# Decays, keys and receptance of a pair of heads loaded in one transfer of 128 rows instead of one per head

## The chip, the cores and the metric

The kernel runs on one core of a Trainium2 chip. Its engines are TensorE (PE, matrix products), VectorE (DVE), ScalarE (ACT), GpSimd (POOL) and SyncE (SP), which here only issues DMAs; 16 DMA engines carry the transfers. The metric is the time of the program on the device in microseconds, the median of several runs.

## The reference

Three parts follow one another. The first is a linear attention with decay, for 4 batches, 8 heads, 768 steps and a head width of 48. The second is a product of gated matrices without a nonlinearity, and the third a mixture of 8 experts, two for each token.

```python
for t in range(S):                                   # per batch and head
    cur = einsum('bhd,bhe->bhde', u[None] * k[t], v[t])
    y[t] = einsum('bhd,bhde->bhe', r[t], state + cur)
    state = w[t][:, None] * state + einsum('bhd,bhe->bhde', k[t], v[t])
x = y as [3072, 384]
x = ((x @ w1) * (x @ w2)) @ w3 @ w_out               # 384 -> 1024 -> 1024 -> 384
logits = x @ w_gate + log1p(exp(x @ w_noise)) * noise
out = sum over the two best experts e: weight * relu(x @ ew1[e]) @ ew2[e]
```

Everything is float32.

## The kernel before

**Stages.** The attention works on pairs of heads: 4 batches of 4 pairs, 16 in all, numbered g = 4 b + q. Three stages follow one another on every engine. In the opening (to about 106 us) the four pairs of batch 0 run, interleaved with the product of w3 and w_out (`w3_mm`: 8 rows of blocks, each with its own load of w3T, 512 KB) and with the preparation of w1 and w2 (loads of wraw, 512 KB, from which w12h and w12l are made). In the middle (to about 478 us) the fused layer of one batch runs beside the attention of the next, and behind it the experts with their own weights.

**A pair.** Its heads share the 128 partitions: head 0 lies in partitions 0 to 47, head 1 in 64 to 111. Rows 48 to 63 and 112 to 127 are fill, 1 for the decays and 0 for keys and receptance, so that every later step may work on all 128. The steps of a pair on DVE are the running product of the decays (`dve_decays`, L254, six scans of wt), its reciprocal (`dve_inverse`, L265, three times), the scaled keys (`dve_keys`, kt, L272) and queries (`dve_queries`, rt, L278), then ruk from the rows kn and rn (L289, L295) and its sums diag (L304). ACT spreads diag into att (L317). PE computes the scores in two halves (L186), turns the scaled keys (L195), forms the products for the state (L207) and the outputs (L231, L237). DVE masks each half of the scores (L325) and steps the state (L335).

**Loads.** All of them are issued by SP, in the order in which its program stands, and go through the same 16 DMA engines. Each tile wt, kt, rt, kn, rn, vs has two buffers. A pair's transposed inputs come from arrays that the host has laid out as [batch, head, 64, 768], already with the fill; `sp_input_load` (L140 to 148) loads one of the three tensors of a pair with two transfers, one for each head. For the first two pairs (g < 2), which fill the two buffers, a transfer has all 64 rows; from then on 48, since the fill rows stay in the buffer. A row has 768 values, 3,072 bytes. So a transfer has 192 KB or 144 KB. The semaphore `loaded` counts 16 per transfer, and DVE waits for 32 per pair. The rows kn and rn (288 KB each) and the values vs (384 KB: 128 rows of 3,072 bytes) have one transfer per pair already.

**The order around the loads.** In the opening SP first issues the loads of pairs 0 and 1 with w_out (two of 768 KB), w3T 0 and 1 and two of wraw between them; the rest follows the list of steps (`order`, made by `threaded`): the loads of pair g + 2 are issued in the place of the same step for pair g + 1, each behind a wait for the buffer (L144), the stores of the attention's output at `out` (L169, four per pair), vs behind them, and w3T n + 2 at the end of block row n (L526). The table of slots (slot_entry, 1,568 KB) is written after the first output of pair 1. PE waits at the first block of each row of w3T for its load (L682), and whatever stands behind this in its program, the second half of a pair's scores among them, waits too.

Of the kernel before, what the change touches and what calls it, by code (L numbers as in the profile page):

```python
# [5 lines left out]
B, H, S, D = 4, 8, 768, 48  # L6
# [8 lines left out]
HP = H // 2  # L15
HB = 64
# [29 lines left out]
def need(eng, sem, count):  # L46

    if not isinstance(count, int) or count > 0:
        eng.wait_ge(sem, count)
# [8 lines left out]
def program(nc, w_turned, k_turned, r_turned, k_rows, r_rows, v_rows, u, w1, w2, w3_turned, w_out, gate_rows, noise_rows, ew1, ew2_rows, out):  # L58
# [10 lines left out]
    with top:  # L69
# [34 lines left out]
        wt, kt, rt = ([asb(f"{x}t{i}", [P, S]) for i in range(2)] for x in "wkr")  # L104
# [19 lines left out]
        loaded = [[sem(f"{x}_loaded{i}") for i in range(2)] for x in "wkr"]  # L124
# [15 lines left out]

        def sp_input_load(sp, b, q, n):
            g, i = HP * b + q, q % 2
            rows = HB if g < 2 else D
            need(sp, (decay_ready, kdiv_ready, rdec_ready)[n], g - 1)  # L144
            for h in range(2):
                sp.dma_start((wt, kt, rt)[n][i][h * HB:h * HB + rows, :],
                             (w_turned, k_turned, r_turned)[n][bass.ds(b, 1), 2 * q + h, 0:rows, :].rearrange("o d t -> (o d) t")
                             ).then_inc(loaded[n][i], 16)

        def sp_rows_load(sp, b, q):  # L150
            g, i = HP * b + q, q % 2
# [96 lines left out]
        def dve_decays(dve, b, q):  # L248

            g = HP * b + q  # L250
            dve.wait_ge(loaded[0][q % 2], 32 * (2 * b + q // 2 + 1))
            need(dve, state_ready, (NC - 1) * (g - 1))
            for c in range(NC):
                last = nc.vector.tensor_tensor_scan(decay[q % 2][:, c, 1:C + 1], wt[q % 2][:, c * C:(c + 1) * C],  # L254
                                                    wt[q % 2][:, c * C:(c + 1) * C], 1.0, ALU.mult, ALU.bypass)
            last.then_inc(decay_ready, 1)
# [10 lines left out]

        def dve_keys(dve, b, q):
            g = HP * b + q
            dve.wait_ge(loaded[1][q % 2], 32 * (2 * b + q // 2 + 1))  # L270
            dve.wait_ge(inverse_ready, 3 * (g + 1))
            nc.vector.tensor_tensor(kdiv[q % 2][:, :], kt[q % 2][:, :], kdiv[q % 2][:, :], ALU.mult).then_inc(kdiv_ready, 1)  # L272

        def dve_queries(dve, b, q):
            g = HP * b + q
            dve.wait_ge(loaded[2][q % 2], 32 * (2 * b + q // 2 + 1))
            need(dve, yu_full, 3 * (g - 1))
            nc.vector.tensor_tensor(rdec[q % 2][:, :].rearrange("p (c x) -> p c x", c=NC),  # L278
                                    rt[q % 2][:, :].rearrange("p (c x) -> p c x", c=NC), decay[q % 2][:, :, 0:C],
                                    ALU.mult).then_inc(rdec_ready, 1)  # L280
# [169 lines left out]
        def sp_attention(sp, b, step, q, n):  # L450

            if later(b, q) is None:
                return
            after = later(b, q + 2)
            b, q = later(b, q)
            g = HP * b + q
            if step == "out":
                sp_attention_store(sp, b, q, n)
                if n == 1 and after:
                    sp_values_load(sp, *after)  # L460
            elif not after:
                return
            elif step == "derive" and n in (0, 4, 5):
                sp_input_load(sp, *after, max(0, n - 3))
            elif step == "diag" and n == 0:
                sp_rows_load(sp, *after)
# [31 lines left out]
        with ExitStack() as ph:  # L498
# [24 lines left out]
            def first_sp(sp):  # L523
# [4 lines left out]
                def load_w12(n):  # L528
# [3 lines left out]
                    sp.dma_start(wraw[n % 2][:, :], (w1, w2)[m][kk * P:(kk + 1) * P, :]).then_inc(wraw_loaded[n % 2], 16)  # L532

                sp_input_load(sp, 0, 0, 0)
                for part in range(2):
                    sp.dma_start(wo[:, 4 * part:4 * part + 4, 0:DM],
# [1147 lines left out]
def laid_out(np, inputs):  # L1684

    a = {name: np.asarray(x) for name, x in inputs.items()}

    def turned(x, fill):
        return np.pad(x.transpose(0, 1, 3, 2), [(0, 0), (0, 0), (0, HB - D), (0, 0)], constant_values=fill)

    def rows(x, pad):
        x = x.reshape(B, HP, 2, NC, P, D).transpose(0, 1, 4, 3, 2, 5)
        return np.pad(x, [(0, 0)] * 5 + [(0, pad)])

    return {
        "w": turned(a["w"], 1), "k": turned(a["k"], 0), "r": turned(a["r"], 0),
        "k_rows": rows(a["k"], 0), "r_rows": rows(a["r"], 0), "v_rows": rows(a["v"], HB - D), "u": a["u"],
        "moe_w1": a["moe_w1"], "moe_w2": a["moe_w2"],
        "moe_w3": a["moe_w3"].reshape(KF, P, KF, P).transpose(0, 3, 2, 1).reshape(KF, P, F1),
        "moe_w_out": a["moe_w_out"],  # L1700
        "gates": np.concatenate([a["moe2_w_gate"], a["moe2_w_noise"]], axis=1).reshape(KD, P, 2 * E).transpose(1, 0, 2),
        "moe2_noise": a["moe2_noise"].reshape(NT, P, E).transpose(1, 0, 2),
        "moe2_w1": a["moe2_w1"],
        "moe2_w2": a["moe2_w2"].reshape(E, KF // 2, 2, P, DM).transpose(0, 1, 3, 2, 4),
    }
# [17 lines left out]
```

## Time and profile before

| | us |
|---|---|
| median of 3 runs | 997.93 (997.01 to 1000.2) |
| the profiled execution, own time | 993.22 |
| its span, first to last instruction | 991.5 |
| PE busy | 951.2 (96%) |
| DVE busy | 676.3 (68%) |
| ACT busy | 528.1 (53%) |
| SP's hardware queue, share of the 16 DMA engines | 50.7% |
| mean granted clock of TensorE | 0.99 of full speed |

Busy times are those of the span. In a table of windows the columns are: the stretch, its length, busy time and instructions of PE, PE's weight loads, DVE, ACT and POOL, then the granted clock, the busy share of the DMA engines and the GB/s that they moved. In a timeline they are start, busy time, engine, line, operation, output and inputs, count, and in brackets the idle time before it with its releaser. SPq is SP's queue of DMA issues: the time there is that of the issue, not of the transfer.

### The profile page before, as it was taken

Reading aid. Unit: us, or ns where it says so; the run is one execution under the profiler, and the core shown is the slowest. Engines: PE = TensorE matmul, PEld = TensorE weight load, DVE = VectorE, ACT = ScalarE, POOL = GpSimd, SP = SyncE. Lnnn points to the kernel's source line nnn. Section 1 sums busy time; section 2 is a strip of 40 time slices with the busy share of each in tenths; the row PEclk is TensorE's granted clock in tenths of the full one; section 3 lists DMA queues with packets and bytes.
Section 4 is the critical chain, followed back from the end, with each engine's and each line's share of the span. In section 5 each row is a group of like instructions: output and inputs, shape, how many; then the busy total and the mean of one; then the engine's idle time right before and its main releaser. Section 6 shows DMA issues by size and latency. Waiting matters only on the chain.

```text
span 991.5 us, 18086 instructions
## 1 busy us (share of the span) xinstructions
PE 951.2 (96%) x6825; PEld 895.8 (90%) x6825; DVE 676.3 (68%) x1133; ACT 528.1 (53%) x986; POOL 221.3 (22%) x209
## 2 busy tenths in 40 slices
PE   5799999999999999999989999999999999999995
PEld 3455899999999999999989999999999999999995
DVE  5688886969696966256766685656856558566570
ACT  3354454555454645325644575655756557565560
POOL 0000000020202020221443323344232432324311
PEclk9889999999999999999999999999999999999998
DMA  9968434353435121216548797877968779787751
GB/s 262 295 190 263 142 85 143 105 160 95 143 106 172 57 71 41 81 52 217 177 123 244 196 294 214 241 257 205 308 206 243 262 202 301 211 245 258 212 152 17
DMA packets 93771, 179.61 MB, mean 181 GB/s; under 512 B 19042, under 2 KB 50532, under 8 KB 93684
## 3 DMA queue, kind: packets, MB, share of 16 engines
q1 hardware_dynamic: 80308, 157.77, 50.7%
q0 software_dynamic: 12976, 20.66, 10.1%
q8 instruction: 54, 0.88, 0.4%
q14 instruction: 33, 0.27, 0.1%
q10 hardware_dynamic: 400, 0.02, 0.0%
HBM read 152.81 MB, written 26.97 MB: 181 GB/s over the span
## 4 chain that ended last, share of the span: by engine, by line
PE 86%; DVE 3%; DMA 3%; ACT 2%; SPq 2%; issue 2%; another core or an unknown queue 0%; POOL 0%; DVEq 0%; ACTq 0%; POOLq 0%
PE pp L1233 20%; PE bank L1217 19%; PE bank L788 13%; PE bank L805 7%; PE fx L788 6%; PE fx L805 4%; PE yu L1276 3%; PE pp L186 2%; DMA w3T<-in_moe_w 2%; PE tr L1198 2%; PE yu L1258 1%; PE fx L1258 1%; PE yu L207 1%; PE yu L237 1%; DMA rn<-in_r_rows 1%
## 5 line engine op out<-in xcount | busy, mean ns | idle before, releaser
L1127 POOL DMA_INDIRECT result<-x2s,who x55 | 92.4, 1681 | 292.5 <-ACT x2s L1350 279.6
L1337 DVE SCALAR_TENSOR_TENSOR abl<-bank,abh 128x512 fp32r<-128x512 f32 x96 | 66.2, 691 | 113.7 <-ACT abh L1332 90.0
L978 POOL DMA_INDIRECT slot_entry<-entry,slot_i x48 | 52.1, 1086 | 334.6 <-DVE token_f L967 322.4
L1217 PE MATMUL bank<-xh,set_up_h 128*128 128x256 f32 x384 | 109.2, 284 | 0.0
L1217 PE MATMUL bank<-xh,set_up_l 128*128 128x256 f32 x384 | 108.6, 283 | 0.0
L1217 PE MATMUL bank<-xl,set_up_h 128*128 128x256 f32 x384 | 108.6, 283 | 0.0
L1332 ACT ACTIVATE abh<-bank 128x512 fp32r<-128x512 f32 x96 | 57.5, 599 | 85.1 <-PE bank L1217 80.2
L788 PE MATMUL bank<-xh,w12h 128*128 128x384 f32 x264 | 89.5, 339 | 1.0 <-DVE xl L485 0.9
L788 PE MATMUL bank<-xh,w12l 128*128 128x384 f32 x264 | 88.4, 335 | 0.0
L788 PE MATMUL bank<-xl,w12h 128*128 128x384 f32 x264 | 88.2, 334 | 0.0
L1233 PE MATMUL pp<-set_down_h,abh 128*128 128x384 f32 x256 | 87.7, 342 | 0.0
L1233 PE MATMUL pp<-set_down_h,abl 128*128 128x384 f32 x256 | 85.7, 335 | 0.0
L1233 PE MATMUL pp<-set_down_l,abh 128*128 128x384 f32 x256 | 85.6, 334 | 0.0
L265 DVE RECIPROCAL kdiv<-decay 128x256 f32<-128x256 f32 x48 | 82.2, 1734 | 0.3
L1114 POOL DMA_INDIRECT tokens<-ffn_out,who x55 | 72.6, 1319 | 32.9 <-issue 23.3
L1217 PEld LDWEIGHTS bank<-xh,set_up_h 128*128 128x128 f32 x384 | 73.5, 191 | 0.5 <-DVE abl L1337 0.2
L1217 PEld LDWEIGHTS bank<-xl,set_up_h 128*128 128x128 f32 x384 | 73.5, 192 | 0.3
L1217 PEld LDWEIGHTS bank<-xh,set_up_l 128*128 128x128 f32 x384 | 73.5, 191 | 0.0
L1350 ACT ACTIVATE x2s<-pp,who 128x384 f32<-128x384 f32 x48 | 28.0, 582 | 84.3 <-PE pp L1233 75.5
L317 ACT ACTIVATE att<-ident,diag 128x128 f32<-128x128 f32 x192 | 59.4, 389 | 15.0 <-DVE diag L304 15.0
L1305 DVE TENSOR_TENSOR set_up_l<-up_raw,set_up_h 128x1024 fp32r<-128x1024 f32 x48 | 57.6, 1224 | 9.3 <-ACT set_up_h L1300 8.8
L1305 DVE TENSOR_TENSOR w12l<-up_raw,w12h 128x1024 fp32r<-128x1024 f32 x45 | 55.0, 1223 | 8.5 <-ACT w12h L1300 5.6
(254 smaller groups left out, 2646.2 us busy)
## 6 DMA issues: line engine op xcount, KB each, us to landing
up_raw<-in_moe_w SPq DMA_DIRECT2D x93, 512.0 KB
down_raw<-in_moe_w SPq DMA_DIRECT2D x124, 384.0 KB
vs<-in_v_rows SPq DMA_DIRECT2D x16, 384.0 KB, 3.6
kn<-in_k_rows SPq DMA_DIRECT2D x16, 288.0 KB, 3.6
rn<-in_r_rows SPq DMA_DIRECT2D x16, 288.0 KB, 4.8
attention_out<-yt SPq DMA_DIRECT2D x64, 72.0 KB, 2.0
result<-zeros SPq DMA_DIRECT2D x12, 384.0 KB
ffn_out<-x2s SPq DMA_DIRECT2D x8, 576.0 KB
```

The source lines that it names most:

```text
L265: nc.vector.reciprocal(kdiv[q % 2][:, :].rearrange("p (c x) -> p c x", c=NC)[:, two, :], decay[q % 2][:, two, 1:C + 1]).then_inc(inverse_r ...
L317: last = nc.scalar.activation(att[:, j, h, c, :], ident[:, :], ACT.Copy, scale=diag[:, 3 * j + c, h:h + 1])
L788: last = nc.tensor.matmul(half_bank[n % 3][:, 0:TG], wp[:, m, kk, f * P:(f + 1) * P], xp[:, kk, :], start=(p == 0), stop=(p == 3 * KD - 1))
L805: last = nc.tensor.matmul(sum_at[s][:, 0:WA], xp[:, f, s * P:(s + 1) * P], wp[:, f, :], start=(f == 0 and n == 0), stop=(f == KF - 1 and n ...
L978: nc.gpsimd.indirect_dma_start(slot_entry, bass.IndirectOffsetOnAxis(slot_i[:, s, n:n + 1], 0), entry[:, s, n, :], None).then_inc(scattere ...
L1114: nc.gpsimd.indirect_dma_start(xg[v % 2][:, s, :], None, stored, bass.IndirectOffsetOnAxis(who[v % 4][:, s, 0:1], 0)).then_inc(gathered[v ...
L1127: nc.gpsimd.indirect_dma_start(out, bass.IndirectOffsetOnAxis(who[v % 4][:, s, 0:1], 0), yo[v % 2][:, s, 0:DM], None, bounds_check=N - 1, ...
L1217: last = nc.tensor.matmul(bank[m % 2][:, f * T2:(f + 1) * T2], wp[:, kk, c:c + P], xp[:, kk, :], start=(n == 0), stop=(n == 3 * KD - 1))
L1233: last = nc.tensor.matmul(pp[:, s, 0:DM], xp[:, f, s * P:(s + 1) * P], wp[:, f, :], start=(f == 0 and n == 0), stop=(f == KF - 1 and n == 2))
L1305: nc.vector.tensor_tensor(low, src, high.bitcast(f32), ALU.subtract).then_inc(w_low, 1)
L1332: nc.scalar.activation(hh[:, 2 * m:2 * m + 2, :].rearrange("p a t -> p (a t)"), bank[m % 2][:, :], ACT.Relu).then_inc(hh_ready, 1)
L1337: nc.vector.scalar_tensor_tensor(hl[:, 2 * m:2 * m + 2, :].rearrange("p a t -> p (a t)"), bank[m % 2][:, :], 0.0, hh[:, 2 * m:2 * m + 2, : ...
```

## The change

`sp_input_load` issues one transfer for a tensor of a pair: all 128 rows, for every pair. The host's arrays are the same bytes, seen as [batch, pair, 128, 768], so that the two heads and their fill lie in one piece. DVE waits for 16 per pair instead of 32. For the 14 pairs from g = 2 on each tensor's transfer carries 32 more rows, 98,304 bytes; for the first two pairs the bytes are the same.

```diff
         def sp_input_load(sp, b, q, n):
             g, i = HP * b + q, q % 2
-            rows = HB if g < 2 else D
             need(sp, (decay_ready, kdiv_ready, rdec_ready)[n], g - 1)
-            for h in range(2):
-                sp.dma_start((wt, kt, rt)[n][i][h * HB:h * HB + rows, :],
-                             (w_turned, k_turned, r_turned)[n][bass.ds(b, 1), 2 * q + h, 0:rows, :].rearrange("o d t -> (o d) t")
-                             ).then_inc(loaded[n][i], 16)
+            sp.dma_start((wt, kt, rt)[n][i][:, :],
+                         (w_turned, k_turned, r_turned)[n][bass.ds(b, 1), q, :, :].rearrange("o x t -> (o x) t")
+                         ).then_inc(loaded[n][i], 16)
...
         def dve_decays(dve, b, q):
-            dve.wait_ge(loaded[0][q % 2], 32 * (2 * b + q // 2 + 1))
+            dve.wait_ge(loaded[0][q % 2], 16 * (2 * b + q // 2 + 1))
...
         def dve_keys(dve, b, q):
-            dve.wait_ge(loaded[1][q % 2], 32 * (2 * b + q // 2 + 1))
+            dve.wait_ge(loaded[1][q % 2], 16 * (2 * b + q // 2 + 1))
...
         def dve_queries(dve, b, q):
-            dve.wait_ge(loaded[2][q % 2], 32 * (2 * b + q // 2 + 1))
+            dve.wait_ge(loaded[2][q % 2], 16 * (2 * b + q // 2 + 1))
...
     def turned(x, fill):
-        return np.pad(x.transpose(0, 1, 3, 2), [(0, 0), (0, 0), (0, HB - D), (0, 0)], constant_values=fill)
+        x = np.pad(x.transpose(0, 1, 3, 2), [(0, 0), (0, 0), (0, HB - D), (0, 0)], constant_values=fill)
+        return x.reshape(B, HP, 2 * HB, S)
```

No engine's instructions change their order. On SP, from its second issue to the loads of pair 0's rows, this stands in a row before (partitions x elements, x how many):

```order
L146 DMA wt<-in_w 64x768 x2
L536 DMA wo<-in_moe_w_out 128x4x384 x2
L146 DMA kt<-in_k 64x768 x2
L146 DMA rt<-in_r 64x768 x2
L526 DMA w3T<-in_moe_w 128x1024
L154 DMA kn<-in_k_rows 128x576
L154 DMA rn<-in_r_rows 128x576
```

and this now:

```order
L144 DMA wt<-in_w 128x768
L534 DMA wo<-in_moe_w_out 128x4x384 x2
L144 DMA kt<-in_k 128x768
L144 DMA rt<-in_r 128x768
L524 DMA w3T<-in_moe_w 128x1024
L152 DMA kn<-in_k_rows 128x576
L152 DMA rn<-in_r_rows 128x576
```

Three issues fewer stand ahead of rn, with the same bytes. Further on in SP's program, from the loads of pair 2 to the third load of w3T, this stands before:

```order
L146 DMA wt<-in_w 48x768 x2
L146 DMA kt<-in_k 48x768 x2
L146 DMA rt<-in_r 48x768 x2
L154 DMA kn<-in_k_rows 128x576
L154 DMA rn<-in_r_rows 128x576
L146 DMA wt<-in_w 48x768 x2
L154 DMA kn<-in_k_rows 128x576
L154 DMA rn<-in_r_rows 128x576
L169 DMA attention_out<-yt 48x3x128 x4
L161 DMA vs<-in_v_rows 128x768
L526 DMA w3T<-in_moe_w 128x1024
```

and this now:

```order
L144 DMA wt<-in_w 128x768
L144 DMA kt<-in_k 128x768
L144 DMA rt<-in_r 128x768
L152 DMA kn<-in_k_rows 128x576
L152 DMA rn<-in_r_rows 128x576
L144 DMA wt<-in_w 128x768
L152 DMA kn<-in_k_rows 128x576
L152 DMA rn<-in_r_rows 128x576
L167 DMA attention_out<-yt 48x3x128 x4
L159 DMA vs<-in_v_rows 128x768
L524 DMA w3T<-in_moe_w 128x1024
```

Four of the loads there (three of pair 2, the decays of pair 3) are one issue instead of two and carry 128 rows instead of twice 48.

## Rows read from the trace of the kernel before

**Rows 1.** The page: tenths in 40 slices, PE busy and granted clock
```profile
PE   5799999999999999999989999999999999999995
PEclk9889999999999999999999999999999999999998
```

**Rows 2.** Windows: the opening, the middle, and a stretch within the opening
```profile
0.00:106.00 106.00, 82.14 (x568) 51.28 (x568) 78.66 (x115) 48.35 (x121) 4.16 (x51) 0.94 0.84 244
106.00:478.00 372.00, 371.29 (x2825) 353.61 (x2826) 273.74 (x612) 180.57 (x448) 42.90 (x40) 1.00 0.37 111
...
55.00:65.00 10.00, 9.79 (x65) 5.67 (x63) 9.97 (x12) 5.01 (x14) 0.00 (x0) 0.95 0.52 157
```

**Rows 3.** The chain that ended last, opening: start us, us, what
```profile
7.79 10.19 DMA rn<-in_r_rows
...
35.99 10.29 DMA w3T<-in_moe_w
...
70.48 10.28 DMA w3T<-in_moe_w
```

**Rows 4.** DMA issues, the w3T issued at 88.63: KB, us to landing
```profile
w3T<-in_moe_w SPq DMA_DIRECT2D x1, 512.0 KB, 5.6
```

**Rows 5.** Windows: stretches in which transfers of one form pass
```profile
26.00:29.50 3.50, 3.50 (x36) 2.03 (x36) 3.36 (x11) 1.46 (x5) 0.00 (x0) 1.00 1.02 404
...
9.00:12.50 3.50, 2.83 (x12) 2.21 (x12) 3.50 (x3) 1.76 (x3) 0.00 (x0) 1.00 1.05 219
18.50:23.50 5.00, 3.71 (x33) 2.23 (x25) 3.04 (x5) 3.44 (x12) 0.00 (x0) 1.00 1.05 234
29.50:34.00 4.50, 4.50 (x32) 2.88 (x27) 4.47 (x5) 1.45 (x3) 0.00 (x0) 1.00 1.05 208
```

**Rows 6.** Windows: the same with their tails, and the slow clock
```profile
9.00:14.50 5.50, 4.73 (x21) 3.88 (x22) 4.05 (x4) 2.35 (x4) 0.00 (x0) 1.00 1.03 241
18.50:26.00 7.50, 5.86 (x65) 4.00 (x58) 4.16 (x7) 5.01 (x16) 0.00 (x0) 1.00 1.04 245
...
29.50:38.00 8.50, 8.03 (x42) 4.59 (x36) 8.36 (x9) 4.95 (x13) 0.00 (x0) 1.00 1.05 224
...
42.50:56.00 13.50, 9.69 (x42) 5.87 (x43) 4.26 (x12) 2.84 (x7) 0.00 (x0) 0.50 0.59 166
```

**Rows 7.** Timeline of SP's issues: the first, and two groups of four stores
```profile
0.82 1.22 SPq L146 DMA_DIRECT2D wt<-in_w  x2
...
32.29 3.17 SPq L169 DMA_DIRECT2D attention_out<-yt  x4
...
118.05 1.81 SPq L169 DMA_DIRECT2D attention_out<-yt  x4
```

**Rows 8.** Timeline, ACT: the first spreads of diag
```profile
20.44 3.62 ACT L317 ACTIVATE att<-ident,diag 128x128 f32<-128x128 f32 x12 [1.23 <-DVE diag L304]
```

**Rows 9.** Timeline, PE and DVE: around the two waits for w3T
```profile
39.50 0.77 PE L195 MATMUL tr<-ident,kdiv 128*128 128x128 f32 x5
...
46.31 3.04 PE L682 MATMUL fx<-wo,w3T 128*128 128x400 f32 x4 [6.05 <-DMA w3T<-in_moe_w]
...
51.05 1.01 DVE L325 COPY_PREDICATED att<-causal,pp 128x768 f32<-128x768 int32 x1 [9.24 <-PE pp L186]
...
52.61 1.18 DVE L335 SCALAR_TENSOR_TENSOR added<-added,decay 128x48 f32<-128x48 f32 x4 [0.55 <-ACT added L341]
...
66.89 1.51 PE L682 MATMUL bank<-wo,w3T 128*128 128x400 f32 x4
...
69.38 1.01 DVE L325 COPY_PREDICATED att<-causal,pp 128x768 f32<-128x768 int32 x1 [1.26 <-PE pp L186]
...
70.42 1.18 DVE L335 SCALAR_TENSOR_TENSOR added<-added,decay 128x48 f32<-128x48 f32 x4
...
80.80 4.30 PE L682 MATMUL bank<-wo,w3T 128*128 128x400 f32 x12 [1.35 <-DMA w3T<-in_moe_w]
...
82.66 0.95 DVE L278 TENSOR_TENSOR rdec<-rt,decay 128x768 f32<-128x768 f32 x1
```

## The prediction

> **What bounds the kernel now.** I read the page first, for the stage that can move. Of 40 slices TensorE (PE) has a busy digit below 9 only in the first two and in the last, and the granted clock has its 8s in the second and third [rows 1]. The table by stage says it in us: from 106 to 478 PE works 371.29 of 372.00 us, in the first 106 only 82.14, with the DMA engines at a share of 0.84 [rows 2]. Behind 478 nothing of the change is left, and between 106 and 478 its loads are issued two pairs ahead of their use, with the DMA engines at 0.37, under a full PE: there I cost the change at nothing. Its cover is that distance, some 50 us, against transfers of under 2 us. So the question is the opening.
>
> The chain of waits runs there through three landings: rn, 10.19 us to 17.98, a w3T, 10.29 us to 46.27, and another, 10.28 us to 80.75 [rows 3]. PE stood 6.05 and 1.35 us for these two w3T, and VectorE (DVE) 9.24 us for the scores that PE computes behind the first [rows 9]. A load of 512 KB that takes 10.3 us, where one issued at 88.63 takes 5.6 [rows 4], stands in a queue. So the next view is the rate of the DMA engines in the stretches that the order of SP's issues lets me name. All 16 are at a share of about 1 in each of the stretches, yet move very different amounts: 404 GB/s in 26.0:29.5, where wraw, vs and wraw pass, all of 128 rows; 219 in 9.0:12.5 (kt and rt of pair 0, halves of 64 rows), 234 in 18.5:23.5 (pair 1), 208 in 29.5:34.0 (pair 2, halves of 48 rows) [rows 5]. Which transfers pass is read by adding up the bytes that SP issues, in its order, against what the engines moved. A half at a time moves at about half speed: that is what the opening pays.
>
> **The change, part by part.** *Rate.* The new transfer is 128 rows of 3,072 bytes in one piece, exactly the form of vs, so I take 404 GB/s. The Trainium skill speaks against that figure: DMA: Bandwidth & Descriptors, "Where 436 GB/s comes from", says that a load from HBM is bound at some 358 GB/s on the HBM side. This trace disagrees (404 GB/s over 3.5 us, [rows 5]); by the page a transfer would take 1.10 us and not 0.97, and the ten ahead of the first w3T 1.3 us more, which the slack of 3 us found below would swallow. The skill's page SBUF — State Buffer, "Can I just issue two DMAs to hit both halves?", gives two concurrent halves only 6% more than one half; if instead they did fill both sides, the merge would save nothing, and the rows (208 to 234 against 404) side with the page.
>
> *Time of the DMA engines ahead of the w3T that PE waits for.* I cut the busy stretches around the slow transfers, with the tail in which they still hold engines up [rows 6], and refill them at 404 GB/s. 9.0:14.5 holds 241 x 5.5 = 1.33 MB: 3.3 us instead of 5.5, saves 2.2. 18.5:26.0 holds 1.84 MB: 4.6 instead of 7.5, saves 2.9. 29.5:38.0 holds 1.90 MB, and four transfers in it (three of pair 2, the decays of pair 3) now carry 32 more rows each, 0.098 MB, in all 0.39: 2.30 MB take 5.7 instead of 8.5, saves 2.8. For the first one, in the start-up, I take 0.9: one issue of 0.6 us falls away ahead of its landing ([rows 7]: two take 1.22), and of its 0.393 MB the rate saves up to 0.393/219 - 0.393/404 = 0.8, of which I count 0.3, as the start-up limits it too. Sum 8.8 us: what was through at 38 is through by 29 or so, before SP issues more.
>
> *A, the start of the chain.* Decays start 0.9 earlier, and rn, for which DVE waits, lands 0.9 + 2.2 = 3.1 earlier, so diag could be ready 3.1 us sooner. ScalarE's spreads, which wait for it, start at 20.44 after an idle time of 1.23 [rows 8]: their engine is free at 19.21, after gates_side, which hangs on wo and moves by the 0.9 only. So they start at 18.3, and the chain gains 2.1 us. Bounds: 1.2 (wo does not move) to 3.1 (all of rn).
>
> *B, the stall for w3T.* Its issue stands behind four stores, which took 3.17 us in the crowded queue and 1.81 in a free one [rows 7]: issue at 35.99 - 2.1 - 1.4 = 32.5. With the queue nearly empty it lands 5.6 us later, or up to 1.3 more with vs and the stores before it: 38.1 to 39.4, I take 38.8. PE is ready for it when its key transposes end (39.50 + 0.77, less 2.1: 38.2) [rows 9]. The wait of 6.05 becomes 0.6: 5.45 us. Bounds 3.0 (as much again queued) to 6.05.
>
> *C, the clock.* From 42.5 to 56 the granted clock is 0.50, the lower of the two levels, after PE had been idle since 40.27 [rows 6, 9]; the pause of 1.35 us before 80.80 saw no fall (the fourth digit is 9, [rows 1]). With a pause of 0.6 us I expect none. From w3T's first matmul to DVE's mask of the second scores the slow stretch took 51.05 - 46.31 = 4.74 us, the same steps at full clock 69.38 - 66.89 = 2.49; from there to DVE's state step 1.56 against 1.04 [rows 9]. Saves 2.25 + 0.5 = 2.8. PE's later matmuls there gain too, but DVE is then busy without a gap to 65 us (9.97 of 10 us from 55) [rows 2] and sets the pace. Bounds 0 to 2.8.
>
> *D, the second stall.* PE waits 1.35 us at 80.80 for w3T. Ahead of it lie kt and rt of pair 4 (two issues fewer, about 1 us of SP; about 0.6 us each of the DMA engines) and the table of slots, which starts earlier. The wait goes; next in line is DVE's rdec (82.66 + 0.95 = 83.6, [rows 9]), so PE's scores, which follow the twelve matmuls begun at 80.80, can move by those 1.3 us and not by more. Bounds 0 to 1.4.
>
> Sum: 2.1 + 5.45 + 2.8 + 1.3 = 11.7 us. From 85 on DVE and PE run as before and carry it to the end. The profiled run goes from 993.22 to 981.5 (span 991.5 to 979.8). The median of the runs, 997.93, lies 4.7 above the profiled run; I take the same 11.7 off it: **986.2**. About 0.3% (3.0 us) is what a measurement of this kernel can tell from no change.
>
> **The rivals.** *The clock falls anyway, or w3T still comes late.* Without C the gain is 8.9 (989.0); with B at its low end too, A at 1.2 and D at 0 it is 4.2 (993.7). For it: w3T's issue hangs on SP's waits, and PE had little to do ahead of it. Against: the queue is empty by then, by 3 us and more. 0.24.
>
> *Hidden anyway.* DVE, busy 78.66 of 106 us, takes over where PE's waits go, or the transfers' rate is set by something that vs escapes and the gain is no more than the saved issues (A at 1.2, and some of the stores' 1.4): 995 to 998. Against: DVE's own largest idle time, 9.24 us at 51.05, is the same stall. 0.07.
>
> *Slower: more bytes at the old rate.* If the merged transfer moved at 208 GB/s, each filled one would cost 0.098 MB / 208 = 0.47 us more: four ahead of the first w3T 1.9, two ahead of the one at 80.75 another 0.95, in all 2.8: 1000.8. It decides below 277 GB/s, where 0.393 MB take as long as 0.295 MB now at 208. For it: only that no row shows this very tensor in 128 rows. Against: vs, whose form it is. 0.03.
>
> *More than summed*: the stalls at 37.5 and 69.4, where PE and DVE pass work back and forth, shrink as well, over 14 us, under 984: 0.03.
>
> **How the numbers follow.** The forecast (9 to 14 us gained) has 0.63. Faster by over 0.3%: 0.63 + 0.24 + 0.03 = 0.90; within 0.3%: 0.07; slower 0.03. The range runs from the sum of the upper ends (13.3, and 0.9 for the spread of the runs: 983.7) to the late end of the first rival, 993.7, and 0.8 more: 983.5 to 994.5; it leaves out the last three cases.
>
> **What would show it.** Right: DMA stretches around kt and rt at 350 GB/s or more; a busy DMA stretch that ends some us before w3T is issued at 32 to 34, landing in under 7 us; no wait over 2 us of PE for w3T; granted clock 1.00 from 42 to 56; the step to the fused layer's first matmul (105.97 now) near 94; the stages behind it as long as before. Wrong: 128-row loads of w, k, r under 277 GB/s; w3T landing after 41; a clock of 0.50 in spite of a short wait; or a stretch behind 106 that is longer by the extra 2.9 MB.

## The result and the profile after

| | before | after |
|---|---|---|
| median of 4 runs, us | 997.47 (993.61 to 1000.2) | 982.92 (980.96 to 983.7) |
| ratio, 95% interval | | 0.9854 (0.9818 to 0.9890) |
| profiled execution, own time | 993.22 | 980.96 |
| its span | 991.5 | 979.2 |
| first matmul of the fused layer (end of the opening) | 105.97 | 93.70 |

The kernel is 14.6 us faster by the medians and 12.3 us by the profiled executions. The forecast said 986.2 in a range from 983.5 to 994.5; the direction, the place and the profiled execution came out (981.5 forecast, 980.96 measured), the median lies 0.6 us under the range.

The page of the kernel after, beside [rows 1], tenths in 40 slices:

```profile
PE   6989999999999999999989999999999999999995
...
PEclk9999999999999999999999999999999999999998
```

The table of windows of the kernel after, by stage, beside [rows 2]:

```profile
0.00:93.70 93.70, 78.75 (x568) 49.75 (x568) 78.51 (x115) 48.34 (x121) 4.16 (x51) 0.96 0.85 291
93.70:465.70 372.00, 371.25 (x2824) 353.57 (x2825) 273.75 (x611) 180.52 (x448) 42.81 (x40) 1.00 0.38 119
465.70:979.20 513.50, 497.81 (x3436) 491.02 (x3434) 323.89 (x408) 299.17 (x418) 175.79 (x118) 0.99 0.74 219
```

Only the first row has changed its length, by 12.27 us. VectorE (DVE) is busy there for 78.5 us, where it was for 78.7; TensorE (PE) for 78.75 instead of 82.14 with the same 568 instructions, at a mean granted clock of 0.96 instead of 0.94. The other two rows are as long as before to 0.1 us, with 119 instead of 111 GB/s in the middle: the 2.9 MB more cost nothing there.

The rates, beside [rows 5]: windows of the kernel after in which kt and rt of pair 0 pass, and those of pairs 1 and 2 among others:

```profile
7.00:9.50 2.50, 2.50 (x13) 2.08 (x13) 2.50 (x2) 1.21 (x3) 0.00 (x0) 1.00 1.06 396
14.00:20.00 6.00, 4.31 (x35) 2.89 (x35) 2.92 (x5) 3.98 (x14) 0.00 (x0) 1.00 1.03 411
26.00:29.00 3.00, 3.00 (x47) 2.36 (x40) 2.97 (x4) 0.96 (x2) 0.00 (x0) 1.00 1.06 401
```

The stretches of 208 to 234 GB/s around these loads are gone; in the three windows the engines move 396 to 411. (Not everything does: in 29.5:34.0 of the kernel after, where the four stores of the attention's output, 48 partitions each, pass with kn, rn and vs, it is 320 GB/s.) From here on w3T 2 is the third load of w3T, the one that PE stood 6.05 us for; the spreads are ScalarE's (ACT's) first ones of diag. The timeline of the kernel after at the places of [rows 8, 9] (start, busy us, in brackets the idle time before):

```profile
6.55 5.12 PE L656 MATMUL bank<-ident,wo 128*128 128x128 f32 x24 [6.55 <-DMA wo<-in_moe_w_out]
...
16.31 3.62 ACT L315 ACTIVATE att<-ident,diag 128x128 f32<-128x128 f32 x12 [2.02 <-DVE diag L302]
...
35.83 0.77 PE L193 MATMUL tr<-ident,kdiv 128*128 128x128 f32 x5
36.43 1.51 PE L680 MATMUL fx<-wo,w3T 128*128 128x400 f32 x4
...
38.93 1.02 DVE L323 COPY_PREDICATED att<-causal,pp 128x768 f32<-128x768 int32 x1 [0.77 <-PE pp L184]
39.97 1.18 DVE L333 SCALAR_TENSOR_TENSOR added<-added,decay 128x48 f32<-128x48 f32 x4
...
56.74 1.02 DVE L323 COPY_PREDICATED att<-causal,pp 128x768 f32<-128x768 int32 x1 [1.26 <-PE pp L184]
57.78 1.18 DVE L333 SCALAR_TENSOR_TENSOR added<-added,decay 128x48 f32<-128x48 f32 x4
...
71.07 0.94 PE L184 MATMUL pp<-rdec,kdiv 48*128 48x128 f32 x12 [1.67 <-DVE kdiv L270]
...
77.76 1.18 DVE L333 SCALAR_TENSOR_TENSOR added<-added,decay 128x48 f32<-128x48 f32 x4
```

PE's wait of 6.05 us for w3T at 46.31 has become none: 36.43 follows straight on the key transposes that begin at 35.83. DVE's wait of 9.24 us for the second scores is 0.77. By DVE's state steps the gain over the kernel before is 3.9 us at the first pair (25.91 to 22.04), 12.6 at the second (52.61 to 39.97) and third (70.42 to 57.78), 14.0 at the scores of the fourth (85.03 to 71.07), and 12.3 at its state step (90.03 to 77.76), where it stays. The rows of before for the first and the last three of these, which stand in no group above:

```profile
25.91 1.18 DVE L335 SCALAR_TENSOR_TENSOR added<-added,decay 128x48 f32<-128x48 f32 x4 [0.43 <-ACT added L341]
...
85.03 0.94 PE L186 MATMUL pp<-rdec,kdiv 48*128 48x128 f32 x12
...
90.03 1.18 DVE L335 SCALAR_TENSOR_TENSOR added<-added,decay 128x48 f32<-128x48 f32 x4
```

The clock in the kernel after:

```profile
20.50:24.50 4.00, 3.94 (x25) 2.56 (x26) 3.20 (x10) 1.91 (x7) 0.00 (x0) 0.57 1.03 405
72.50:75.50 3.00, 3.00 (x8) 1.47 (x6) 1.27 (x2) 0.69 (x1) 0.00 (x0) 0.50 0.61 187
```

The long stretch at the lower level behind the stall (13.5 us, [rows 6]) is gone, but there are two short ones where the kernel before had none. The second lies between the two places at which the gain is 14.0 and 12.3; the 1.7 us between them are put down to it, as PE's five transposes and four matmuls, 0.77 and 1.51 us at full clock (35.83 and 36.43), take 1.22 and 2.79 there (71.94 and 72.95), together 1.7 more.

### The profile page after: what moved, and what is told of

Its sections match the earlier page's. It is cut to its first block, busy times and chain, and to the rows that moved or that the text cites. A ratio compares the mean times of both kernels' runs of the same rounds, so it can differ in the third digit from the quotient of the medians.

```text
span 979.2 us, 18038 instructions
## 1 busy us (share of the span) xinstructions
PE 947.8 (97%) x6825; PEld 894.3 (91%) x6825; DVE 676.2 (69%) x1133; ACT 528.0 (54%) x986; POOL 222.8 (23%) x209
## 3 DMA queue, kind: packets, MB, share of 16 engines
q0 software_dynamic: 12976, 20.66, 10.2%
## 4 chain that ended last, share of the span: by engine, by line
PE 87%; DVE 5%; ACT 3%; issue 2%; DMA 1%; SPq 0%; another core or an unknown queue 0%; POOL 0%; DVEq 0%; ACTq 0%; POOLq 0%
PE pp L1231 20%; PE bank L1215 20%; PE bank L786 13%; PE bank L803 7%; PE fx L786 6%; PE fx L803 4%; PE yu L1274 3%; PE pp L184 3%; PE tr L1196 2%; PE yu L1256 1%; PE fx L1256 1%; PE yu L205 1%; PE yu L235 1%; PE tr L193 1%; DVE kdiv L263 1%
## 5 line engine op out<-in xcount | busy, mean ns | idle before, releaser
L1125 POOL DMA_INDIRECT result<-x2s,who x55 | 92.5, 1681 | 290.3 <-ACT x2s L1348 277.4
L1335 DVE SCALAR_TENSOR_TENSOR abl<-bank,abh 128x512 fp32r<-128x512 f32 x96 | 66.2, 691 | 113.7 <-ACT abh L1330 97.5
```

The costliest lines, as they stand in the source:

```text
L1125: nc.gpsimd.indirect_dma_start(out, bass.IndirectOffsetOnAxis(who[v % 4][:, s, 0:1], 0), yo[v % 2][:, s, 0:DM], None, bounds_check=N - 1, ...
L1335: nc.vector.scalar_tensor_tensor(hl[:, 2 * m:2 * m + 2, :].rearrange("p a t -> p (a t)"), bank[m % 2][:, :], 0.0, hh[:, 2 * m:2 * m + 2, : ...
```

## The experiments

The experiments ran on four chips (4, 5, 12 and 14; that of the first comparison is not on record). Each is compared with runs of the kernel before on its own chip; the start of the expert stage differs from chip to chip (below), so spans are not compared across chips, but openings are.

**What makes the rate: bytes, number, size or partitions?** Two kernels have the bytes of the kernel after in two transfers per tensor. One takes the halves of the kernel before:

```diff
-            sp.dma_start((wt, kt, rt)[n][i][:, :],
-                         (w_turned, k_turned, r_turned)[n][bass.ds(b, 1), q, :, :].rearrange("o x t -> (o x) t")
-                         ).then_inc(loaded[n][i], 16)
+            for h in range(2):
+                sp.dma_start((wt, kt, rt)[n][i][h * HB:(h + 1) * HB, :],
+                             (w_turned, k_turned, r_turned)[n][bass.ds(b, 1), q, h * HB:(h + 1) * HB, :].rearrange("o x t -> (o x) t")
+                             ).then_inc(loaded[n][i], 16)
```

> The kernel after, but each tensor of a pair again in two transfers, rows 0 to 63 and rows 64 to 127, for every pair: the bytes of the kernel after, the number and the halves of the kernel before. Theory (a transfer to one half of the partitions moves at about half the rate): DMA rate around kt and rt of pair 0 near 220 GB/s, w3T 2 lands as late as before or later (46 to 49 us), PE waits 6 us or more for it, the fused layer's first matmul at 106 to 109 us, time 997 to 1001. Rival (the gain comes from something else, such as the layout of the host's arrays or the count of waits): opening ends near 94, time near 983.

The other takes the even rows to the even partitions and the odd ones to the odd:

```diff
-                sp.dma_start((wt, kt, rt)[n][i][h * HB:(h + 1) * HB, :],
-                             (w_turned, k_turned, r_turned)[n][bass.ds(b, 1), q, h * HB:(h + 1) * HB, :].rearrange("o x t -> (o x) t")
+                sp.dma_start((wt, kt, rt)[n][i][h:P:2, :],
+                             (w_turned, k_turned, r_turned)[n][bass.ds(b, 1), q, h:P:2, :].rearrange("o x t -> (o x) t")
```

> As the run with two halves, but one transfer has the even rows and partitions and the other the odd ones: still two issues of 64 rows and 192 KB per tensor, the same bytes, but each transfer spreads over all partitions. Theory (what counts is which partitions one transfer reaches): rate around kt and rt of pair 0 at 350 to 410 GB/s, first matmul of the fused layer at 94 to 97 us (the extra issues cost up to 2 us of SP at the start), time 982 to 987. By the Trainium skill, SBUF - State Buffer, section on the DMA port swizzle, even and odd partitions reach all 16 ports each, which points the same way. Rival (what counts is that the transfer is large and in one piece of DRAM, or that there are fewer issues): rate near 220, opening as before (106), time 997 to 1000.

Measured, with halves: 994.91 us, ratio 1.0030 (1.0004 to 1.0056), opening 111.1 us. Interleaved: 979.58 us, ratio 0.9867 (0.9844 to 0.9890), opening 96.2. Windows around the loads of pairs 0 and 1, halves first:

```profile
10.00:13.00 3.00, 2.72 (x12) 2.10 (x11) 2.41 (x2) 1.41 (x3) 0.00 (x0) 1.00 1.05 239
20.00:24.50 4.50, 2.13 (x7) 0.68 (x4) 2.44 (x5) 2.40 (x9) 0.00 (x0) 0.89 1.03 226
```

and interleaved:

```profile
9.00:12.00 3.00, 1.78 (x9) 1.59 (x9) 2.38 (x2) 0.58 (x1) 0.00 (x0) 1.00 1.03 402
16.00:20.00 4.00, 3.03 (x41) 1.92 (x42) 2.47 (x4) 1.46 (x5) 0.00 (x0) 1.00 1.03 411
```

PE's wait for w3T with halves:

```profile
52.52 3.03 PE L681 MATMUL fx<-wo,w3T 128*128 128x400 f32 x4 [9.74 <-DMA w3T<-in_moe_w]
```

Bytes, number of transfers and size are the same in both; what differs is which rows a transfer takes, and with them its partitions, and the rate goes from 226 to 239 GB/s to 402 to 411. It is neither the single transfer nor one contiguous piece of DRAM: the interleaved transfers read every other row. The two were not tried apart: no run sends the same rows of DRAM to other partitions. That the partitions decide is the reading that fits. The Trainium skill, SBUF — State Buffer, "Door 1: The DMA port swizzle (why `[64,N]` ≈ `[32,N]`)", lets partitions 0 to 63 reach 8 of 16 ports at some 218 GB/s; the windows with halves, in which other loads pass too, lie a little above at 226 to 239. The same page of the Trainium skill, in "Can I just issue two DMAs to hit both halves?", holds that "the only way to hit all 16 ports is one transfer spanning all 128 partitions". The runs part from it if that is read as all 128 in one: transfers of 64 partitions each, spread over both sides, come to 402 to 411 GB/s here. The run with halves is also nearly the slower rival of the prediction, made real (with two issues where the rival has one): the fill rows at the old rate cost 0.30%, 3.0 us, where 2.8 was worked out. The interval of that cost goes from 0.4 to 5.6 us, so its sign is shown and its size is not.

The openings came as expected with interleaved rows (94 to 97) and longer than expected with halves (106 to 109; w3T 2 landed at 52.5, not at 46 to 49). Both times lie below what was expected, 997 to 1001 and 982 to 987: the kernel before takes 992.62 on chip 5, 5 us less than in the first comparison. One thing stays unexplained: with interleaved rows w_out lands later than in the kernel before (PE's first transpose at 10.22 instead of 8.95), although the decays ahead of it are in 1.1 us sooner (their second transfer at 4.25 instead of 5.36 us) and SP issues w_out at the same time.

**Which of the loads pay?** The form of the load is chosen by pair (MERGED is the condition; the waits count 16 or 32 for each pair accordingly):

```diff
+            if MERGED(g):
                 sp.dma_start((wt, kt, rt)[n][i][:, :],
...
+            else:
+                for h in range(2):
+                    sp.dma_start((wt, kt, rt)[n][i][h * HB:h * HB + rows, :],
```

Pairs 0 and 1 merged, the others with 48 rows a head:

> One transfer of 128 rows for the first two pairs only, where it carries the same bytes; from the third pair on two of 48 rows as in the kernel before. Theory: nearly the whole gain at the start (ScalarE's first spreads at 16.3 to 17 us instead of 20.4), but pair 2 and the decays of pair 3 again take 1.5 us each of the DMA engines; since those were through at 29 with a margin, w3T 2 still lands within 2 us of when PE wants it. First matmul of the fused layer at 94 to 97, time 983 to 986. Rival (each of the ten transfers ahead of w3T 2 is needed): w3T 2 is waited for by 2 to 4 us and the clock falls long: 988 to 992.

Pairs 0 and 1 in halves of 64 rows, the others merged:

> Two transfers of 64 rows for the first two pairs, one of 128 from the third pair on. Theory: the start stays as before (ScalarE's first spreads at 20.4 us), the DMA queue is 2.8 us shorter ahead of w3T 2, which lands at 42 to 44 instead of 46.3; PE waits 2 to 4 us for it; the clock falls or not. First matmul of the fused layer at 99 to 103, time 990 to 995. Rival (the stall depends only on the large transfers behind): no change from the kernel before, 997.

Merged from pair 6 on only:

> One transfer of 128 rows only from the seventh pair on, whose loads are issued at the end of the opening and in the middle stage; the first six pairs as in the kernel before (64 and 48 rows a head). Theory: nothing, the middle stage runs at the pace of TensorE; its length stays within 0.5 us of 372, opening ends where that of the kernel before does (104 to 109 us), ratio 1.000 within its interval. Rival (2.9 MB more in the middle stage cost, or faster loads there gain): 1 us or more either way in the middle stage.

| merged | median, us | ratio (interval) | first spreads | wait for w3T 2 | end of opening |
|---|---|---|---|---|---|
| pairs 0, 1 | 980.85 | 0.9883 (0.9857 to 0.9909) | 16.39 | 3.06 | 96.9 |
| from pair 2 | 986.68 | 0.9956 (0.9925 to 0.9987) | 20.54 | 0.35 | 100.8 |
| from pair 6 | 990.92 | 0.9994 (0.9970 to 1.0018) | 20.81 | 5.64 | 107.0 |

PE's wait for w3T 2 in the timeline of the first of the three:

```profile
39.27 3.04 PE L690 MATMUL fx<-wo,w3T 128*128 128x400 f32 x4 [3.06 <-DMA w3T<-in_moe_w]
```

of the second:

```profile
41.87 1.61 PE L690 MATMUL fx<-wo,w3T 128*128 128x400 f32 x4 [0.35 <-DMA w3T<-in_moe_w]
```

and of the third:

```profile
46.28 3.04 PE L690 MATMUL fx<-wo,w3T 128*128 128x400 f32 x4 [5.64 <-DMA w3T<-in_moe_w]
```

Merging the first two pairs moves the start of the chain by 4 us and leaves a wait of 3.06 us, as the rival said and not the theory; the clock fell in it, but only for some 7 us (36.5 to 43.5), and the opening ends where the theory had it. The time lies below both, 983 to 986 and 988 to 992. Merging from the third on leaves the start as it was and takes nearly the whole stall, where 2 to 4 us were expected to stay; the opening came as expected (99 to 103), the time below it (990 to 995). There w3T 2 is issued at 35.99 as in the kernel before and lands in 5.84 us instead of 10.29: 4.4 us saved where the sum had 2.8 for the four transfers ahead of it. Whether the rest comes from kt and rt of pair 3, which follow right behind w3T and are merged too, was not tried apart. By the ratios the first two pairs alone take 1.17%, the others alone 0.44%, together 1.6 where the whole change gives 1.47: within the intervals they add up, though both act on the same stall. From pair 6 on the form is worth nothing that shows: in the middle stage PE works 371.3 of 372 us as before. That cost at nothing held.

**Why did the start gain 4.1 us and not 2.1?** PE's first transpose, which waits for w_out, moved by 2.4 us instead of 0.9. The rows of before:

```profile
8.95 2.88 PE L658 MATMUL bank<-ident,wo 128*128 128x128 f32 x12 [8.95 <-DMA wo<-in_moe_w_out]
12.60 2.91 PE L658 MATMUL bank<-ident,wo 128*128 128x128 f32 x12 [0.77 <-DMA wo<-in_moe_w_out]
```

Keys and receptance of pair 0, which are issued behind w_out, again in two halves of 64 rows, all else as in the kernel after:

```diff
+def MERGED(g, n):
+    return g > 0 or n == 0
```

> The kernel after, but keys and receptance of pair 0, and they alone, in two transfers of 64 rows. They are issued behind w_out. The prediction moved w_out by 0.9 us, it moved by 2.4 (PE's first transpose from 8.95 to 6.55 us). Theory 1 (slow transfers issued behind another hold up its landing): the first transpose starts at 7.5 us or later although nothing ahead of w_out differs from the kernel after, and the second half of the transposes has a gap again. Theory 2 (it is the decays ahead of w_out alone): first transpose at 6.5 us, 24 transposes without a gap to 11.7. In both, rn lands 2 us later than in the kernel after and the spreads start at 17.5 to 18.5 us.

```profile
6.63 4.30 PE L666 MATMUL bank<-ident,wo 128*128 128x128 f32 x20 [6.63 <-DMA wo<-in_moe_w_out]
11.10 0.65 PE L666 MATMUL bank<-ident,wo 128*128 128x128 f32 x4 [0.17 <-ACT woT L590]
```

984.13 us, ratio 0.9861 (0.9827 to 0.9895), spreads at 17.54. The second theory holds for the landing that the first transpose waits for: with the decays in one transfer and the slow ones behind, the first of w_out's two transfers lands at 6.49 us, in the kernel after at 6.41. The second lands 0.6 us later (9.22 instead of 8.61), which PE does not feel. In every profile with the decays in one transfer the first transpose comes at 6.5 to 7.3 us, in every one with two at 8.5 to 10.2.

What it is in the decays is not shown. Their rate it can't be alone: the run with interleaved rows has them in at the full rate, in two transfers, and has the latest w_out of all:

```profile
10.22 5.58 PE L657 MATMUL bank<-ident,wo 128*128 128x128 f32 x24 [10.22 <-DMA wo<-in_moe_w_out]
```

One issue instead of two lets SP issue w_out at 1.27 instead of 2.08 us, 0.8 of the 2.4; the rest is that its first transfer then takes 5.1 us to land instead of 6.7. The spreads come 1.2 us later than in the kernel after since rn lands later (ruk starts at 15.17 instead of 13.44); the expected start of 17.5 to 18.5 holds. The opening ends at 96.4, 3 us later than in the kernel after on that chip, with three falls of the clock (at 17, 54.5 and 75 us); the medians differ by 1.0 us.

**Does filling PE's waits keep the clock up?**

```diff
             if j == 0:
+                if 2 <= g < HP:
+                    pe.wait_ge(tr_free, g)
+                    for c in range(8):
+                        nc.tensor.transpose(tr[:, c // 4, (c % 4) * C:(c % 4 + 1) * C], ident[:, :], ident[:, :])
                 pe.wait_ge(kdiv_ready, g + 1)
```

> The kernel after with eight more transposes of the identity on TensorE ahead of its wait for the keys of pairs 2 and 3, into a PSUM tile that is overwritten next (work that nobody needs, some 1.1 us in a wait of 1.7 to 2.5 us). Theory: the half clock at 72.5 to 75.5 us in the kernel after follows the waits around 69 to 71 us, and cost 1.7 us between the scores of pair 3 (gain over before 14.0 at 71.07, 12.3 at 77.8): with the engine busy there the clock stays at 1.00 and the fused layer starts at 92 to 92.5 us, 1.2 to 1.7 us earlier. Rival (the falls come whatever the engine does in those waits): a fall at the same place, start at 93.7 or later.

982.94 us, beside 983.15 for the kernel after on the same chip. The opening lies between what the theory (92 to 92.5) and the rival (93.7 or later) had. There is no fall at 72, but one at 53.5, and one in the expert stage that this profile has and the kernel after's has not, the first row here, beside the kernel after on the same chip, the second:

```profile
495.19:525.19 30.00, 27.06 (x190) 26.65 (x189) 19.97 (x28) 14.87 (x21) 14.15 (x10) 0.94 0.68 172
```

```profile
495.43:525.43 30.00, 27.10 (x197) 26.70 (x196) 22.53 (x32) 17.61 (x25) 13.21 (x9) 1.00 0.75 201
```

Opening 93.2 against 93.4. That filling these waits avoids a fall is not shown, nor that it moved this one: a third profile of the unchanged kernel has no fall at 72 either. Over three profiles of the kernel after the falls lie at 20.5 and 72.0, at 71.5, and at 52.5 us: executions of one kernel differ in them.

**Can the start be shortened further?** In the kernel after DVE waits 0.54 us for the vector u of the reference (u_all), and the spreads for what follows. w3T 0 is issued behind kn, rn and u instead of ahead of them:

```diff
-                load_w3(0)
                 sp_rows_load(sp, 0, 0)
                 sp.dma_start(u_all[:, :, :, :].rearrange("p q h d -> p (q h d)"),
                              bass.AP(u.tensor, u.offset, [[0, P], [1, H * D]])).then_inc(small_loaded, 16)
+                load_w3(0)
```

> The kernel after with w3T 0 issued behind kn, rn and u of pair 0 instead of ahead of them. In the kernel after VectorE waits 0.54 us for u, and ScalarE's spreads wait 2.0 us for the diag that follows. Theory: rn and u land 1.3 us earlier (524 KB at 400 GB/s), spreads start at 15.5 to 15.7 instead of 16.3, w3T 0 lands before TensorE wants it at 16.6; opening ends 0.6 to 0.8 us earlier unless the clock falls elsewhere, time about 0.7 us under the kernel after. Rival (w3T 0 now comes late, or a fall of the clock eats it): same time or up to 1 us longer.

978.05 us beside 976.77 for the kernel after on the same chip. The spreads start at 15.47, as expected. The opening ends at 93.1 instead of 95.5, or 93.4 and 93.7 in the other two profiles of the kernel after; but the clock falls right behind it, at 93, and the stages behind take 883.4 us instead of 881.5. No gain that a measurement shows.

**How far do executions of one kernel differ?** Both kernels, unchanged, once more, and the kernel before in three further executions:

> The kernel before, unchanged, with a profile of its own on the chip of the other experiments. Its runs there spread from 983.7 to 997.5 us, those of the merged kernels only over some 3 us. Theory: everything that differs between executions of the kernel before lies in the opening (when w3T 2 lands, whether and how long the clock falls behind it); this profile has its first matmul of the fused layer between 98 and 108 us, and everything behind it takes the same as in the other profiles of this chip (882 us). Rival: the spread lies in the expert stage, which would differ by several us from the other profiles.

> The kernel after, unchanged, on the chip of the other experiments, so that it can be compared with them. Theory: opening ends at 93 to 95 us as in its first profile, time 975 to 980, below the run with interleaved halves (979.6) by the 2.5 us that its opening is shorter. Rival (it has no advantage over interleaved halves, clock and landings even it out): 979 to 981.

> The kernel after once more, beside the run with u ahead of w3T and for a third profile of its opening: 93 to 94 us with one or two falls of the clock, ratio to the kernel before 0.985 to 0.987.

> The kernel before, unchanged, for one more profiled execution. Its runs spread over 8 to 14 us on each chip, those of the kernel after over 3. Theory 1: the spread is in the opening and goes with how long the clock stands at its lower level there; behind the opening everything takes the same to 0.5 us. Theory 2: it is the landing of the first loads, that is the start of the spreads (20.4 and 21.0 us in two profiles) and w3T 2 (46.3, 47.4). Each profile tells the two apart by where its difference to the others arises.

> As b_look1, another execution: the same two theories; an execution with a long opening should show it either at the start of the spreads and w3T 2, or in later steps where the clock fell once more.

> As b_look1, another execution of the unchanged kernel before: the same two theories, told apart by the step at which its opening parts from the others.

| kernel, profile | chip | span | first spreads | w3T 2 starts | opening | behind it |
|---|---|---|---|---|---|---|
| before, first | | 991.5 | 20.44 | 46.31 | 105.97 | 885.5 |
| before, again | 4 | 994.0 | 20.99 | 47.42 | 108.48 | 885.5 |
| before, third | 12 | 995.3 | 22.06 | 48.65 | 108.19 | 887.1 |
| before, fourth | 12 | 995.7 | 21.67 | 48.47 | 107.50 | 888.2 |
| before, fifth | 12 | 990.8 | 20.39 | 48.16 | 105.55 | 885.2 |
| after, first | | 979.2 | 16.31 | 36.43 | 93.70 | 885.5 |
| after, again | 4 | 979.0 | 16.27 | 36.08 | 93.43 | 885.6 |
| after, third | 14 | 977.0 | 16.57 | 36.80 | 95.48 | 881.5 |

The kernel after again: 983.15 us on chip 4, ratio 0.9853 (0.9826 to 0.9881), and 976.77 on chip 14, ratio 0.9851 (0.9823 to 0.9878), against 998.10 and 991.35 for the kernel before there. Ten further runs of the kernel before on chip 4: 995.59, ratio 0.9986 (0.9958 to 1.0014). What was expected of these runs missed in part: the kernel after took 983.15 where 975 to 980 were expected, and the stages behind the opening 885.5 where 882 were, both figures of chip 5 where the runs were on chip 4; the openings of 108.48 and 95.48 lie above 98 to 108 and 93 to 94. Whether the kernel after is faster than the one with interleaved halves, as its opening says (93.4 to 95.5 us against 96.2), its ratios don't show: 0.9853 and 0.9851 against 0.9867, with overlapping intervals.

The runs: on chip 4 the kernel before took 990.3 to 1001.7 us in 13 runs, the four shortest at a mean clock of 0.988 to 0.991, the four longest at 0.983 to 0.988; the kernel after 980.8 to 983.8, all at 0.993. Neither of the two theories stands alone. The openings of the kernel before part by 1.7 us already at the first spreads (20.39 to 22.06), that is with the landing of the early loads, and by 2.9 at their end, with falls of the clock at different places. And there is a third place: behind the opening, at the start of the experts, where the third and the fourth profile had a fall of the clock and the fifth not:

```profile
510.19:540.19 30.00, 27.06 (x187) 26.66 (x187) 21.21 (x30) 16.25 (x23) 11.75 (x9) 0.94 0.71 189
```

```profile
507.55:537.55 30.00, 27.15 (x196) 26.74 (x196) 22.61 (x32) 17.81 (x25) 12.97 (x9) 1.00 0.77 203
```

(windows of 30 us at the same distance behind the opening; the first row is the third profile, the second the fifth, at full clock). Where the longest runs, up to 1001.7, lose their time is not seen: none of the profiled ones was over 995.7 in span.

## Why the prediction was right or wrong

The median lies 3.3 us under the forecast. 2.3 of them are the step from the profiled execution to the median, which took the distance between the two to be the same for both kernels; 0.6 are the sum, 12.3 instead of 11.7; the rest is a fourth run of the kernel before, by which its median is 997.47 and not 997.93. Within the sum the term that failed is the 0.9 us for the first load, in A. The rate, the queue and the stall were right. Two readings of [rows 1] are not quite so: PE's digit is 8 in the 21st slice too, and the granted clock's in the last. Both lie behind the middle stage, and nothing hangs on them.

**The rate and the queue: right.** 404 GB/s was taken, 396 to 411 were measured. The 358 GB/s of the Trainium skill (DMA: Bandwidth & Descriptors, "Where 436 GB/s comes from"), which were weighed against it, are passed here too, by 411 GB/s over 6 us. w3T 2 was issued at 30.94 (32.5 forecast) and landed in 5.1 us (5.6 to 6.9).

```profile
w3T<-in_moe_w SPq DMA_DIRECT2D x1, 512.0 KB, 5.1
```

**A, the start: 4.1 us, not 2.1.** The step that failed is "gates_side, which hangs on wo and moves by the 0.9 only" (gates_side is ScalarE's copy of the product of w_out and the gates, ahead of the spreads in its program). w_out moved by 2.4 and PE's transposes lost their gap as well, so gates_side ended at 14.28 and not at 18.3. The error is the 0.9 for the first load, and it is the same 1.5 us twice: w_out came 2.4 earlier instead of 0.9, and rn landed 4.6 earlier (17.97 to 13.35) instead of 3.1, so that even the bound of 3.1 was passed. The run with only kt and rt in halves shows that the form of the decays' load is worth the 2.4 us. Why it is worth more than the issue saved, 0.8 us, stays open; that the engines are held up by the slow rate of the halves, the term of which I counted 0.3, does not explain it, as the run with interleaved rows shows. Of the chain it was then u, not gates_side, that set the start, which the sum didn't have:

```profile
13.91 0.37 ACT L588 COPY gates_side<-fx 128x256 f32<-128x256 f32 x1 [1.62 <-PE fx L665]
...
14.73 0.76 DVE L293 TENSOR_TENSOR ruk<-ruk,u_all 128x576 f32<-128x576 f32 x1 [0.54 <-DMA u_all<-in_u]
```

**B, the stall: 6.05 us, not 5.45.** No wait is left in the first profile (w3T landed at 36.0, PE took it at 36.43), 0.40 us in the third: just in time, as summed.

**C, the clock: right where the stall was, wrong as a whole.** B and C together gave 8.8 us between the first and the second state step (26.70 before, 17.93 after), where 8.25 were summed. But "with a pause of 0.6 us I expect none" held for that place only. The clock fell at 20.5 us (the gain of 4.1 us at the spreads is 3.9 at the first state step) and at 72.

**D, the second stall: 1.3 us gained, then 1.7 lost.** The scores of pair 3 came 1.3 us earlier relative to the step before, as summed, limited by rdec as said: they start at 71.07, when rdec ends (70.02 + 0.95); the keys that their row names were done at 70.10. Then the fall at 72 took 1.7 us, so D's net is -0.4. The rival of a clock that falls anyway was right in kind and smaller than priced.

The errors nearly cancel: 1.8 more in A by the first state step, 0.5 more in B and C, 1.7 less in D: 12.3 instead of 11.7. That the profiled execution came within 0.6 us of the forecast is in part luck.

**The median: the step that put it outside.** "The median of the runs lies 4.7 above the profiled run; I take the same 11.7 off it" takes the distance between a run and its median as a property of both kernels. It was one of the kernel before, whose profiled execution was a quick one, 4.3 us under the median of the four runs; in the kernel after the distance is 2.0. So the medians part by 14.6 us and the profiled executions by 12.3. The runs of the kernel before spread by 7 to 14 us on the chips on which it ran more than once, in 4 to 19 runs, those of the kernel after by 3, in 4 or 5. Between the two profiles on chip 4, 108.48 and 93.43, the opening differs by 15.0 us, between the two first ones by 12.3; the medians, by 14.6, lie between. What makes the runs of the kernel before spread is only shown in part (above). The range had 0.9 us for the spread of the runs, taken from the distance of the fastest to the median of three, which was far too little for a kernel whose runs lie 3 us apart in three.

**The rivals.** *Slower by more bytes at the old rate* did not come true, since the rate is the one of vs; its price of 2.8 us lies within what the run with halves measured, 0.4 to 5.6. *Hidden anyway* is out: DVE's busy time in the opening stayed, 78.5 us, and the opening became 12.3 us shorter around it. *More than summed* had "under 984", where the median lies, but not for its reason: DVE's wait at the mask after the second stall is 1.26 us in both kernels (69.38 and 56.74), and PE's for the scores' keys grew from 1.1 to 4.2 us in the opening. That its number came is luck. The middle stage cost and gained nothing.

## What to carry to other kernels

Here transfers to partitions 0 to 63 or 64 to 127 alone moved at about half the rate (208 to 239 GB/s) of those that spread over both sides (396 to 411); look at the GB/s of stretches in which the DMA engines are at a share of 1, and ask of each slow stretch to which partitions its transfers go. Fill rows that make such a transfer whole can be free, as here with a third more bytes. Taking one issue away ahead of the first loads was worth more than the issue itself (2.4 us where 0.8 were saved on SP), which no sum of bytes and rates gave. And before subtracting a profiled gain from a median, ask how far the runs of each kernel spread and whether the stall that is removed is what spreads them.

## What was not expected of the hardware

- Two transfers of 64 rows to even and to odd partitions, from every other row of DRAM, move at 402 to 411 GB/s, as fast as one of 128 rows; two of 64 rows to the two halves, both queued at once on the same 16 engines, at 226 to 239. Two halves that lie in the queue together don't add up to the full rate.
- 411 GB/s from DRAM to SBUF over 6 us.
- Whether the first load is one transfer or two moves the landing of the next by more than the issue: the first transfer of w_out landed 5.1 us after its issue behind one, 6.7 behind two, in the first profiles.
- The clock falls at different places in executions of one kernel (20.5 and 72.0, 71.5, 52.5 us), after waits as short as 1.7 us, where before it stayed up through waits of 1.35 us. Which of the waits it takes was not settled.
- The start of the experts takes 3 to 4 us more in all nine profiles of chips 4 and 12 and of the first comparison than in the seven of chips 5 and 14, whatever the kernel. The difference lies in one place: 404 to 410 us behind the opening PE stands for 2.8 to 2.9 us in two waits for `abl` (L1335 of the kernel after), which are absent in the seven. With that and with falls of the clock and smaller waits it is 885.2 to 888.3 us behind the opening against 881.5 to 883.4. Why it goes by the chip is not known.
